# A fused recurrence and two MLPs on one Trainium2 core: states advanced in one instruction per pair, two weight slots split early with GpSimd held, attention units two steps later

## The reference, cut to what matters

```python
for t in range(S):                                   # S = 768, D = 48
    cur = einsum('bhd,bhe->bhde', u * k_t, v_t)
    y[:, :, t] = einsum('bhd,bhde->bhe', r_t, state + cur)
    state = w[:, :, None] * state + einsum('bhd,bhe->bhde', k_t, v_t)
x = y.transpose(0, 2, 1, 3).reshape(3072, 384)
h = x @ w_in;  x = (maximum(h, 0) + alpha * minimum(h, 0)) @ w_out        # first MLP
h = x @ w_in2; out = (h * tanh(softplus(h))) @ w_out2                     # second MLP
```

## Time and profile before

| | us |
|---|---|
| median of 3 runs | 998.72 (996.91 to 998.73) |
| the profiled execution, its own time | 999.02 |
| its span, first to last instruction | 997.2 |
| TensorE matmuls busy | 964.7 (97%) |
| VectorE busy | 678.7 (68%) |
| ScalarE busy | 619.7 (62%) |
| GpSimd busy | 377.0 (38%) |

### The profile page before, as it was taken

The page is one execution under the profiler, slowest core; times in us unless marked ns, Lnnn a source line. Parts: engine busy times, 40 slices in busy tenths (PEclk is TensorE's granted clock), DMA queues, the critical chain, the costliest instruction groups (busy, mean ns, idle before and its releaser), DMA issues.

```text
span 997.2 us, 23888 instructions
## 1 busy us (share of the span) xinstructions
PE 964.7 (97%) x9476; PEld 794.4 (80%) x9476; DVE 678.7 (68%) x1368; ACT 619.7 (62%) x1272; POOL 377.0 (38%) x663
## 2 busy tenths in 40 slices
PE   4887999999999999999999999999999999999998
PEld 4766778888888888888888888888888888888886
DVE  8987776666656666666653346877777777777775
ACT  5744665544554454555444658878778777787775
POOL 9984779667666676666500440000000000000000
PEclk9957999999999999999999999999999999999999
DMA  6323341212221121111003332100000000000000
GB/s 183 107 57 108 109 139 46 79 46 55 61 77 46 52 86 45 46 45 62 16 11 139 95 95 80 33 1 32 33 33 32 1 32 0 0 32 0 33 1 32
DMA packets 24610, 54.29 MB, mean 54 GB/s; under 512 B 4928, under 2 KB 12736, under 8 KB 24512
## 3 DMA queue, kind: packets, MB, share of 16 engines
q1 hardware_dynamic: 22640, 43.43, 14.9%
q10 hardware_dynamic: 1872, 9.49, 2.4%
HBM read 41.10 MB, written 9.44 MB: 51 GB/s over the span
## 4 chain that ended last, share of the span: by engine, by line
PE 91%; DVE 6%; issue 1%; DMA 1%; ACT 0%; ACTq 0%; SPq 0%; DVEq 0%
PE acc L1005 41%; PE hid L989 29%; PE lev L989 10%; PE lev L1047 7%; DVE scores L596 3%; PE tok L1064 2%; PE tok L1070 2%; DVE arena L307 1%; PE tok L1021 1%; DVE w_lo L681 1%; DMA arena<-rk_t 1%; DVE state L573 0%; ACTq L318 0%; DVE diag L605 0%; DVE x_parts L614 0%
## 5 line engine op out<-in xcount | busy, mean ns | idle before, releaser
L989 PE MATMUL hid<-x_parts,w_hi 128*128 128x512 f32 x864 | 291.2, 391 | 2.6 <-DMA x_parts<-y 1.3
L1005 PE MATMUL acc<-g_hi,w_hi 128*128 128x512 f32 x576 | 231.4, 402 | 0.0
L1005 PE MATMUL acc<-g_hi,w_lo 128*128 128x512 f32 x576 | 225.6, 392 | 0.0
L989 PEld LDWEIGHTS hid<-x_parts,w_hi 128*128 128x128 f32 x864 | 163.0, 189 | 37.9 <-issue 1.7
L596 DVE COPY_PREDICATED scores<-mask,lev 64x128 f32<-64x128 int8 x420 | 149.6, 356 | 29.9 <-ACT scores L841 18.2
L989 PE MATMUL hid<-x_parts,w_lo 128*128 128x512 f32 x432 | 168.9, 391 | 0.0
L879 ACT ACTIVATE relu_neg<-hid 128x512 f32<-128x512 f32 x96 | 57.3, 597 | 176.7 <-PE hid L989 174.8
L1005 PE MATMUL acc<-g_lo,w_hi 128*128 128x512 f32 x576 | 162.3, 390 | 0.0
L687 DVE SCALAR_TENSOR_TENSOR hid<-relu_neg,neg_slope,hid 128x512 f32<-128x512 f32 x96 | 72.5, 755 | 120.1 <-ACT hid L880 119.9
L1005 PEld LDWEIGHTS acc<-g_hi,w_hi 128*128 128x128 f32 x576 | 108.4, 188 | 23.8 <-issue 0.2
L1005 PEld LDWEIGHTS acc<-g_lo,w_hi 128*128 128x128 f32 x576 | 108.3, 188 | 23.1
(11 more groups left out here) (92 smaller groups left out, 1353.4 us busy)
## 6 DMA issues: line engine op xcount, KB each, us to landing
w_raw<-weights SPq DMA_DIRECT2D x32, 384.0 KB, 3.1
arena<-rkv SPq DMA_DIRECT2D x24, 384.0 KB, 3.1
arena<-rk_t SPq DMA_DIRECT2D x48, 192.0 KB, 3.6
arena<-rkv SPq DMA_DIRECT2D x24, 192.0 KB, 2.6
x_dram<-result ACTq DMA_DIRECT2D x6, 768.0 KB, 3.6
arena<-x_dram SPq DMA_DIRECT2D x6, 768.0 KB, 4.3
out<-result ACTq DMA_DIRECT2D x6, 768.0 KB, 3.3
x_parts<-y SPq DMA_DIRECT2D x141, 16.0 KB, 1.9
```

The lines of the kernel that those rows point to most:

```text
L989: last = nc.tensor.matmul(to[:, 0:TILE], w[:, j, kt * P:(kt + 1) * P], x[:, par, kt], start=x is x_hi and w is w_hi and kt == 0, stop=x is ...
L1005: last = nc.tensor.matmul(acc[d][:, 0:TILE], w[:, j, cols], g[:, j % RING], start=j == 0 and g is g_hi and w is w_hi, stop=j == STEPS - 1 ...
```

## The change

It has four parts.
1. `advance_state` uses one SCALAR_TENSOR_TENSOR for each of the four pairs (state times decay, plus the summed bank) where it had two TENSOR_TENSOR instructions over all pairs with a wait between them.
2. `EARLY` goes from 2 to 3: `split_lo(1)` and `split_lo(2)` stand on VectorE behind the diagonal sum of unit 8, ahead of pick(9). In `tile1` slot j+3 is split at step j instead of slot j+2. ScalarE's `split_hi` moves in the same way, with slot 3 ahead of `copy_high(7)`. GpSimd waits in chunk 5, between its keys and its queries, until three slots are split on VectorE.
3. Scores, attends, sums and states of `tile1` move to later steps: attend(9) to step 1, score(10) to step 2, attend(10) and score(11) to step 4, and so on, and `advance_state` moves up ahead of the step's low part. The last unit is attended at step 78. On GpSimd `split_lo` of slots 6, 10 and 14 stands ahead of `rows_for_state`.
4. Of the six hole DMAs of chunk 3, SyncE issues four and ScalarE two (three and three before).

```diff
-EARLY = 2
+EARLY = 3
@@
         def unit_at(s):
 
-            v = FIRST + s // 2
-            return v if s % 2 == 0 and v < UNITS else None
+            v = FIRST - 1 + s // 2
+            return v if s % 2 == 0 and s > 0 and v < UNITS else None
+
+        def attended_at(s):
+
+            v = FIRST - 2 + s // 2
+            return FIRST - 1 if s == 1 else v if s % 2 == 0 and FIRST <= v < UNITS else None
 
         def chunk_ended_at(s):
 
-            v = FIRST + s // 2
-            return v // PER_CHUNK - 1 if s % 2 == 0 and v % PER_CHUNK == 0 and v <= UNITS else None
+            v = attended_at(s)
+            return v // PER_CHUNK if v is not None and v % PER_CHUNK == PER_CHUNK - 1 else None
 
         def chunk_summed_at(s):
 
-            c = (s + 19) // 4
-            return c if s % 4 == 1 and c < CHUNKS else None
+            c = (s + 17) // 4
+            return c if s % 4 == 3 and c < CHUNKS else None
@@ SyncE
-            fill_holes(sp, CHUNKS_PER_TILE - 1, (0,))
+            fill_holes(sp, CHUNKS_PER_TILE - 1, ((1, 0), (0, 0), (0, 1), (0, 2)))
@@ GpSimd, chunk()
                 keys_of(c, par, 0)
+                if isinstance(c, int) and c == CHUNKS_PER_TILE + 1:
+                    pool.wait_ge(wlo_dve, EARLY)
                 queries_of(c, par, 0)
                 scale_for_state(c, par, uses)
-                rows_for_state(c, par, 0)
                 for i in slots:
                     split_lo(i)
+                rows_for_state(c, par, 0)
@@ VectorE, advance_state()
-                nc.vector.tensor_tensor(new, now, spread(w_pow[0:ROWS, LEVELS], 2, D), ALU.mult).then_inc(state_done, 1)
                 dve.wait_ge(summed, c + 1 - (c + 1) // PER_SEQUENCE)
-                dve.wait_ge(state_done, 2 * c + 1)
-                nc.vector.tensor_tensor(new, new, bank[0:ROWS].rearrange("p (a n) -> p a n", a=PAIRS)[:, :, 0:D],
-                                        ALU.add).then_inc(state_done, 1)
+                for p in range(PAIRS):
+                    last = nc.vector.scalar_tensor_tensor(new[:, p], now[:, p], w_pow[0:ROWS, LEVELS, p:p + 1],
+                                                          bank[0:ROWS, CHUNK * p:CHUNK * p + D], ALU.mult, ALU.add)
+                last.then_inc(state_done, 2)
@@ VectorE, first_tile()
-                split_lo(1)
+                    if v == FIRST - PER_CHUNK:
+                        for i in range(1, EARLY):
+                            split_lo(i)
@@ VectorE, tile1()
                     activate(s, j)
+                    if summing is not None:
+                        advance_state(summing, tok)
...
-                    if summing is not None:
-                        advance_state(summing, tok)
-                        if summing < CHUNKS - 1:
-                            sum_diagonal(summing + 1, (summing + 1) % 2)
+                    if summing is not None and summing < CHUNKS - 1:
+                        sum_diagonal(summing + 1, (summing + 1) % 2)
@@ ScalarE, first_tile()
-                slot_before = {0: 0, 3: 1, 5: 2}
+                slot_before = {0: 0, 3: 1, 5: 2, 7: 3}
...
-                            fill_holes(act, c - 1, (1,))
-                fill_diagonal(FIRST)
+                            fill_holes(act, c - 1, ((1, 1), (1, 2)))
@@ TensorE, tile1()
-                    if s % 2 == 0 and FIRST + s // 2 <= UNITS:
-                        attend(FIRST + s // 2 - 1, 1)
-                    unit, summing = unit_at(s), chunk_summed_at(s)
+                    attended, unit, summing = attended_at(s), unit_at(s), chunk_summed_at(s)
+                    if attended is not None:
+                        attend(attended, 1)
```

More of the change, by code:

```diff
@@ L23 @@
+import itertools
 import numpy as np
@@ L308, in scale_key_level, with fill_holes @@
                                                          CHUNK // (2 * m)), ALU.mult)
-        def fill_holes(engine, c, halves=(1, 0)):
+        def fill_holes(engine, c, places=tuple(itertools.product((1, 0), range(KT)))):
             odd, cc = c // CHUNKS_PER_TILE % 2, c % CHUNKS_PER_TILE
-            for q in halves:
+            for q, k in places:
                 engine.wait_ge(ylo_done if q else xlo_done, c + 1)
-                for k in range(KT):
-                    first = HALF * q + (HALF - D) * k
-                    holes = x_parts[HALF * q + D:HALF * (q + 1), odd, :, k, cc * CHUNK:(cc + 1) * CHUNK]
-                    engine.dma_start(holes.bitcast(F32), y3[first:first + HALF - D, c % 2].bitcast(F32)
-                                     ).then_inc(holes_in[c % 2], 16)
+                first = HALF * q + (HALF - D) * k
+                holes = x_parts[HALF * q + D:HALF * (q + 1), odd, :, k, cc * CHUNK:(cc + 1) * CHUNK]
+                engine.dma_start(holes.bitcast(F32), y3[first:first + HALF - D, c % 2].bitcast(F32)
+                                 ).then_inc(holes_in[c % 2], 16)
         @block.sync
```

## The result

| | before | after |
|---|---|---|
| median of 5 runs, us | 998.72 (996.91 to 998.87) | 993.24 (991.43 to 993.72) |
| the profiled execution, own time | 999.02 | 993.24 |
| its span | 997.2 | 991.5 |
| TensorE / VectorE / ScalarE / GpSimd busy | 964.7 / 678.7 / 619.7 / 377.0 | 966.5 / 674.4 / 618.4 / 377.0 |

The ratio of after to before is 0.9946, 95% interval 0.9932 to 0.9961: 5.4 us faster. The forecast was 986.0, so it promised 12.7 and less than half came. The time lies 0.24 us outside the range.

The account below looks back on a forecast made before the run. It took the first 92 us, with VectorE delayed by GpSimd, TensorE waits and a fallen clock, as where time was lost. 3.2 + 10.0 - 1.6 + 1.3 - 0.1 = 12.8 us gave 986.0 us, range 983 to 993.

Parts of the forecast that it names:

- state update: advance_state on VectorE: four instructions of 0.6 us in total escape GpSimd's delays; gain 3.2 us, bounds 1.5 and 4.0.
- start of tile: small waits and old wait: TensorE behind up(0): the waits of 0.53 and 0.77 us and the old 4.56 ahead of attend(10) go.
- start of tile: old half-rate stretch: TensorE from 86.89 to about 95.2 us: the half-rate stretch takes half the time, giving back 4.1 us.
- new wait ahead of attend(10): TensorE, ready at 88.65, waits about 1.6 us for pick(10), act(3) and the memset, ending at 90.2.
- clock behind it: TensorE behind the wait ahead of attend(10): clock stays at full, no loss counted.
- state waits: Later chunks: advance_state runs a full step ahead of the attend that needs it; gain 1.3 us.
- tile boundaries: Holes of a tile's last chunk have two steps instead of four; 1.6 us left except at step 80, cost 0.1 us.
- Slots 1 and 2 early: Two splits of 0.9 us on VectorE fill the gap before pick(9), which up(0) does not await; cost nothing.
- "Under the 2.5 us ... before the clock fell": The 1.6 us wait ahead of attend(10) is under the 2.5 us TensorE had idled before the clock fell at some 85.
- The rival "the wait moves and stays long": split_lo(3) meets GpSimd, memset 3 us later, attend(10) waits 4 us or more, clock falls again: 993; chance 0.20.
- The rival of late holes: Tile boundaries: last hole DMA lands 3 us late, TensorE waits 1 to 2 us at each of five; slower, chance 0.05.
- the one in which the clock never falls before up(0): Without VectorE's 2.13 us stall, up(0) may run at full rate and end 2 us earlier: 984; chance 0.10.

Follow-up runs that it names:

- 2.3 alone: Kernel before with only the four state-update instructions in advance_state: 995.02 us, ratio 0.9977 (0.9968 to 0.9987).
- one split in the gap: Changed kernel with EARLY back at 2 and GpSimd's hold kept, so only slot 1 is split early: 988.63 us, ratio 0.9902.
- three splits in the gap: Changed kernel with split_lo(3) also moved into the early gap and GpSimd held for three splits: 988.58 us, ratio 0.9920; again on another chip 988.21, 0.9890.
- load 6 first: Changed kernel with SyncE loading slot 6 ahead of chunk 4's hole DMAs: 991.80 us, ratio 0.9941.
- longer hold: Changed kernel with GpSimd also held until split_lo(3) is done: 995.93 us, ratio 0.9975.
- Relieving both: Changed kernel with split_lo(3) also in the early gap and slot 6 loaded ahead of chunk 4's hole DMAs: 986.62 us, ratio 0.9897.
- the longer hold with load 6 first: Changed kernel with GpSimd held until split_lo(3) is done and slot 6 loaded ahead of chunk 4's hole DMAs: 999.01 us, ratio 1.0011.
- the change again: The changed kernel rerun without edits, on the chip of other runs: 993.29 us, ratio 0.9953.
- the shift alone: Kernel before with only the later attention steps, advance_state moved and GpSimd's splits ahead of rows_for_state: 992.18 us, ratio 0.9951.
- without the hold: Changed kernel without GpSimd's wait for three low parts: 992.52 us, ratio 0.9945.
- shift and state update: Kernel before with the later attention steps and the new state update, without the early splits: 990.75 us, ratio 0.9933.
- early splits only: Kernel before with only the early splits, GpSimd's hold and the moved ScalarE splits and DMAs: 998.19 us, ratio 1.0002.

## Why the prediction was wrong, by its own steps

| term | forecast | measured |
|---|---|---|
| state update | 3.2 | 2.9 at up(0); 2.3 alone |
| start of tile: small waits and old wait | 5.86 | 5.86 |
| start of tile: old half-rate stretch | 4.1 | 3.9 (gone) |
| new wait ahead of attend(10) | -1.6 | -3.2 |
| clock behind it | 0 | -4.6 |
| state waits | 1.3 | 1.3 |
| tile boundaries | -0.1 | -0.4 |
| sum | 12.8 | 5.8 |

The profiled executions differ by 999.02 - 993.24 = 5.8 us, so these terms account for it. Nearly all that is missing stands in two of them, the new wait and the clock behind it.

**State update: right.** Four instructions take 0.78 us, not 0.6, and the gain at up(0) is 2.86, not 3.2. The 0.96 columns per ns behind the 0.6 does not follow from the two rows that it rests on, which differ by 256 columns and 195 ns; but the 0.78 lies within the bounds of 0.5 to 1.1. The Trainium skill (VectorE: DVE Perf Modes, section The TRN2 errata), from which the prediction worked out an estimated 0.83 us and a gain of 2.8, was the nearer of the two. Its advice against short instructions did not decide, since they replace one that GpSimd could stop.

**Slots 1 and 2 early: the instructions right, "cost nothing" wrong.** They ran in 1.82 us, up(0) waited for its holes as before, and the small waits went. But `EARLY` moves every later slot too. I asked of `split_hi(6)` only whether its load would end near pick(10), and kept `split_lo(3)` out of the chain altogether. Both bear on attend(10), and one split in the gap is 4 to 5 us faster than two.

**A new wait of 1.6 us: this is the step that failed.** The prediction reckons this step in the time of the kernel before, with up(0) at 68.77, and takes the gain of the state update off separately: it puts `split_lo(3)` at 76.1, and with up(0) 2.86 us earlier it stood at 73.27. So the times are compared by their distance from the start of up(0):

| us behind the start of up(0) | reckoned | measured |
|---|---|---|
| full clock returns | 5.3 | 5.6 |
| TensorE ready for attend(10) | 19.9 | 20.4 |
| load of slot 6 landed | 18.7 | 20.4 |
| memset done | 21.4 | 23.5 |

TensorE's side was right to 0.5 us. The memset was 2.1 us late, and that is what turned 1.6 us of waiting into 3.2. What the reckoning lacked is the length of the splits beside GpSimd. `split_lo(3)` does not appear in it at all, as if it ended unnoticed in its undisturbed 0.95 us. It took 2.97 us (3.57 and 3.68 in two other profiles of this order), and act(1) behind it started 1.8 us later than its input allowed. `split_lo(5)`, put at 1.2 us, took 1.79. The same 1.8 us went into the load of slot 6 by way of chunk 4's hole DMAs: with three splits in the gap they were issued 9.4 and 9.3 us behind up(0) in place of 11.2. Even then the load landed 19.3 and 19.7 us behind it, 0.5 to 1.0 later than the reckoned 18.7, so it still bound. Relieving one of the two bounds left a wait of 2.1 to 5.7 us (load 6 first, three splits, longer hold). Relieving both left 0.61, and 986.62 us; the longer hold with load 6 first left 1.55, with its load still late.

**"Under the 2.5 us ... before the clock fell": followed from this.** With 3.2 us the clock fell and took 4.6 us. The step from 1.6 to 3.2 us of waiting thus cost 1.6 + 4.6 = 6.2 of the missing 7.0 us. The prediction had named both as signs that it was wrong, a wait over 3 us and matmuls at half rate behind it.

**The rival "the wait moves and stays long" is what happened**, by its mechanism, `split_lo(3)` amid GpSimd's work. I gave it 0.20. Its sizes were too large: it had the memset 3 us later and a wait of 4 us or more, where 2.1 and 3.2 were measured (4.21 in the change again). That its 993 is right to 0.2 us is partly luck. It counted nothing for the old wait and its half-rate stretch, of whose 8.5 us 0.7 were won in fact, and this was offset by the smaller gain of the state update and the wait at step 80. I held the median of 16 splits, 0.95 us, against it. But that median hides that six of the 16 took 1.24 to 4.75 us beside GpSimd, and the one of 4.75 us stood at the same kind of place, the start of the tile.

**State waits and tile boundaries: right.** The former are gone. Of the latter only step 80 waits, 0.4 us. The rival of late holes did not occur, nor the one in which the clock never falls before up(0): it was at 0.50 in the first windows of up(0) here too.

**What stays open.** The rule by which the clock falls is not settled by these runs, and neither is the share of runs in which a split passes GpSimd early, for a profile shows one execution. Why one split gets in among short GpSimd instructions and another stands behind twelve of them is not shown either.

## What to carry to other kernels

An instruction that is moved needs the duration of its new place, not its median over the kernel: the split of 0.95 us took 2.97 where it met GpSimd, and everything behind it moved. When a wait is reckoned, measure both of its sides from one common event, here the start of up(0); only then does it show which side was late. Where several chains end within the same microseconds (here VectorE's order and a weight load), removing one may give little, so edit them together: by the ratios, the load moved alone gave nothing that could be measured, the longer hold alone lost 2 to 3 us, and three splits in the gap with the load first gave 5 to 6. A knob that puts two pieces into a free gap also pulls every later piece forward, so look at where the later ones land.

## What the runs showed of the hardware

**Where a stopped split gets in.** A VectorE instruction with two SBUF operands can stand behind many GpSimd instructions, 10.02 us in the case above. All eleven splits with a row of their own that took over 2.5 us in the profiles of this case (2.55 to 10.02, before and after the change) ended 0.73 or 0.74 us behind the start of the same GpSimd instruction: the one that adds the bonus to `ruk`, L472 here, L466 before, L473 in the kernels with the shift alone or with the state update. That instruction reads what the one ahead of it wrote. Between the two GpSimd pauses by 0.07 to 0.09 us, while its other instructions, where they wait for no other engine, follow without a pause, and then it takes 1.58 to 1.61 us instead of 1.01. So these splits got in at such a pause of GpSimd. Other delayed splits got in elsewhere, most of them within a run of six short products, which then took 3.15 us instead of 2.42; these took 1.0 to 2.1 us. The Trainium skill (SBUF — State Buffer, section Who interferes with whom) says that a tensor_tensor with both inputs in SBUF contends with GpSimd's reads, and calls the shared ports an exclusive lock, which whoever issues first has for the whole instruction (it says this of the 2-port modes). By that a split would stand behind one GpSimd instruction. The rows agree with the first and not with the second: at 93.83 it stood behind sixteen (L482, L461, L455, twelve short products and L468).

**The clock after idle.** Behind up(0), TensorE's waits of 0.61, 1.55 and 1.82 us left the clock full, and so did one of 2.43 us (without the hold). Waits of 2.08, 2.32, 2.50, 3.00 us and all longer ones were followed by half rate. So the same idle time, a little over 2 us, goes either way. Summed over the windows behind the wait, each fall cost between 1.5 us (shift and state update) and 5.0 us (early splits only) of work at full rate. It was more than the wait in some profiles (4.6 against 3.22 in the change) and less in others (1.5 against 4.18 with shift and state update).
